# Half-height matmuls in pairs for a gated two-product layer: nine half passes in the first product, w_out stationary in the second, tiles of 1024 tokens

## What is computed

```python
# attention-like part: x (4, 4096, 192), weight_gen (4, 4096, 8 heads, 7 taps)
w = exp(weight_gen - max over taps);  w = w / (sum over taps + 1e-9)
x_pad = six zero rows ahead of each sequence
out[b, s, h, :] = sum over k of w[b, s, h, k] * x_pad[b, s + k, h, :]     # 24 channels per head
# feed-forward part, on x = out as (16384, 192); w_in (192, 2048), w_out (2048, 192)
h = x @ w_in
g = h * sigmoid(1.702 * h)
return g @ w_out                                                          # (16384, 192), float32
```

## Time and profile before

| what | us |
|---|---|
| median of 3 runs (1236.51 to 1236.57) | 1236.51 |
| the profiled execution's own time | 1236.58 |
| its span in the trace | 1234.8 |
| TensorE busy | 1189.4 (96%) |
| TensorE weight loads busy | 1071.5 (87%) |
| VectorE busy | 876.8 (71%) |
| ScalarE busy | 588.4 (48%) |
| first matmul starts | 36.32 |

### The profile page before, as it was taken

How to read it: one execution, slowest core, us unless ns; L and a number is a source line. 1 busy time by engine, 2 the same in 40 slices (tenths; PEclk the granted TensorE clock), 3 DMA queues, 4 the chain that set the end, 5 groups by cost and what they waited for, 6 DMA issues and landing times.

```text
span 1234.8 us, 17474 instructions
## 1 busy us (share of the span) xinstructions
PE 1189.4 (96%) x6656; PEld 1071.5 (87%) x6656; DVE 876.8 (71%) x1064; ACT 588.4 (48%) x726; POOL 34.2 (3%) x14
## 2 busy tenths in 40 slices
PE   0789999999999999999999999999999999999998
PEld 0678998998998998998998998998998998999998
DVE  7997777777777777777777777777777777777742
ACT  2467454454454454454454454454454454454453
POOL 5320000000000000000000000000000000000000
PEclk9999999999999999999999999999999999999999
DMA  6000000000000000000000000000000000000000
GB/s 273 18 7 25 31 31 30 30 14 16 30 30 30 30 15 15 30 30 30 30 15 16 30 30 30 30 17 14 30 30 30 30 17 14 30 30 30 14 14 13
DMA packets 10670, 37.43 MB, mean 30 GB/s; under 512 B 1312, under 2 KB 1568, under 8 KB 10528
## 3 DMA queue, kind: packets, MB, share of 16 engines
q1 hardware_dynamic: 10368, 36.18, 8.5%
q10 hardware_dynamic: 288, 1.05, 0.2%
HBM read 24.64 MB, written 12.58 MB: 30 GB/s over the span
## 4 chain that ended last, share of the span: by engine, by line
PE 92%; DVE 7%; DMA 1%; ACT 0%; issue 0%; SPq 0%; DVEq 0%
PE acc L411 31%; PE acc L413 15%; PE hid L392 10%; PE hid L393 9%; PE hid L395 9%; PE hid L394 9%; PE hid L396 9%; DVE prod L266 2%; DVE sums L271 1%; DVE gate_lo L333 1%; DVE tap_max L286 1%; DMA xwin<-in_x_runs 1%; DVE sums L266 0%; DVE conv L274 0%; DVE tap_norm L255 0%; DVE turned L297 0%
## 5 line engine op out<-in xcount | busy, mean ns | idle before, releaser
L411 PE MATMUL acc<-w,gate_hi 128*128 128x384 f32 x2048 | 601.0, 357 | 5.5 <-DVE gate_lo L333 4.8
L333 DVE TENSOR_TENSOR gate_lo<-gate,gate_hi 128x1024 fp32r<-128x1024 f32 x256 | 313.8, 1226 | 335.5 <-ACT gate_hi L219 335.5
L216 ACT ACTIVATE gate<-hid 128x1024 f32<-128x1024 f32 x256 | 262.7, 1026 | 604.0 <-PE hid L396 598.5
L413 PE MATMUL acc<-w,gate_lo 128*128 128x192 f32 x2048 | 519.1, 253 | 0.0
L411 PEld LDWEIGHTS acc<-w,gate_hi 128*128 128x128 f32 x2048 | 385.2, 188 | 18.7 <-DVE gate_lo L333 7.1
L413 PEld LDWEIGHTS acc<-w,gate_lo 128*128 128x128 f32 x2048 | 391.2, 191 | 10.7
L219 ACT ACTIVATE gate_hi<-hid 128x1024 fp32r<-128x1024 f32 x256 | 260.8, 1019 | 0.0
L392 PE MATMUL hid<-xt,w_hi 128*128 128x512 f32 x512 | 209.1, 408 | 36.3 <-DVE xt L306 36.3
L393 PE MATMUL hid<-xt,w_hi 128*128 128x512 f32 x512 | 204.7, 400 | 0.0
L395 PE MATMUL hid<-xt,w1r_hi 128*128 128x512 f32 x512 | 203.0, 396 | 0.0
L394 PE MATMUL hid<-xt,w_lo 128*128 128x512 f32 x512 | 202.8, 396 | 0.0
(11 more groups left out here) (27 smaller groups left out, 280.1 us busy)
## 6 DMA issues: line engine op xcount, KB each, us to landing
xwin<-in_x_runs SPq DMA_DIRECT2D x32, 528.0 KB, 3.8
out<-outs SPq DMA_DIRECT2D x32, 384.0 KB, 2.5
taps<-in_tap_runs SPq DMA_DIRECT2D x1, 3248.0 KB, 18.7
w_raw<-in_w_rows SPq DMA_DIRECT2D x2, 768.0 KB, 10.2
w_raw<-in_w_rows ACTq DMA_DIRECT2D x1, 512.0 KB, 4.1
w1r_raw<-in_w1r_rows ACTq DMA_DIRECT2D x1, 512.0 KB, 6.1
w_raw<-in_w_rows SPq DMA_DIRECT2D x1, 512.0 KB, 9.6
w1r_raw<-in_w1r_rows SPq DMA_DIRECT2D x1, 512.0 KB, 10.4
```

The lines of the kernel that those rows point to most:

```text
L216: nc.scalar.activation(gate[:, s, :], hid[:, s, :, :], ACT.Gelu_apprx_sigmoid).then_inc(gate_ready, 1)
L333: nc.vector.tensor_tensor(gate_lo[:, i, :], gate[:, m % 2, :], gate_hi[:, i, :], ALU.subtract).then_inc(gate_lo_ready, 1)
L411: nc.tensor.matmul(acc[:, t, 0:2 * D], gate_hi[:, i, g], w2[:, c, :], start=(c == 0), stop=False)
L413: last = nc.tensor.matmul(acc[:, t, D:2 * D], gate_lo[:, i, g], w2[:, c, 0:D], start=False, stop=(c == CH - 1))
```

## The change

**Tiles.** 64 runs instead of 32. A tile is 1024 tokens in two halves h of 512, and there are 16. 128 partitions hold half h (64 of them each), in it two groups of 96 channels by 32 runs. Each VectorE step of the convolution has 1536 elements a partition for 1024 tokens instead of 768 for 512. After one transposition (three slices k of 32 channels) the channels of half h are on partitions 64h to 64h+63, 64 at a time.

**First product.** A unit is one chunk of 128 hidden columns for each half, 16 units a tile, 256 in all. It makes 3 terms by 3 slices, nine passes; each pass is two matmuls of 64 x 128 weights by 512 tokens, one for each half of the array's rows. The halves' weights come from the upper or lower 64 partitions, and each partition half has at first only half of w_in's columns; four DMAs copy them across before unit 8 of tile 0.

**Second product.** w_out is stationary, the gate moves with 512 columns. The accumulators hold 128 output columns (`acc_main`) and the other 64, hi in the lower and lo in the upper half (`acc_rest`), for each h a bank. A chunk's 128 hidden columns are two half heights, and a bank may take only one half of the array at a time: rows 0-63 go to bank 0 while rows 64-127 go to bank 1 (straight), then the reverse (crosswise), with waits on TensorE's own semaphores at the turns. That is ten passes of two matmuls a unit.

**Around it.** Read-out is one copy each on ScalarE and VectorE for `acc_main`, then ScalarE copies and VectorE adds twice for `acc_rest`, in slot `v == 1`, on VectorE ahead of that unit's `gate_lo`. The output leaves in two stores a tile. `xwin` and the output buffers are single. GpSimd has no work: w_in's and w_out's lo parts and the taps' subtraction are VectorE's. The raw weights lie in the space of the later taps, so these are loaded only after the weights are split.

```diff
+CONV_AT = (4, 0, 2, 1, 1, 2, 1, 1, 2, 1, 1, 1, 0, 0, 0, 0)
+TURN_AT, ROUND_AT, SPLIT_AT = 11, 12, 13
+TAPS_AT = (1, 3, 6, 8)
...
-        xwin = sb("xwin", [P, 2, WIN, CB])
+        xwin = sb("xwin", [P, WIN, CB])
...
             load_taps(0, 0, taps_loaded[0])
+            sp.dma_start(xwin[:], x_runs[:, 0:WIN, :]).then_inc(x_loaded, 16)
+            sp.dma_start(w1_raw, w1_rows).then_inc(w1_loaded, 16)
+            sp.dma_start(w2_raw, w2_rows).then_inc(w2_loaded, 16)
             load_taps(1, 1, taps_loaded[1])
+            sp.wait_ge(w1_hi_ready, 1)
+            sp.dma_start(w1_hi[lower, :, 1, :].bitcast(F32), w1_hi[upper, :, 0, :].bitcast(F32)).then_inc(w1_doubled, 16)
...
+            sp.wait_ge(w2_lo_ready, 2)
+            load_taps(2, 1 + PARTS, taps_loaded[2])
 
             def tile(j, b):
+                if not is_last(j):
                     wait(sp, conv_ready, j + 1)
+                    sp.dma_start(xwin[:], x_runs[:, bass.ds(U * (j + 1), WIN), :]).then_inc(x_loaded, 16)
+                wait(sp, main_out_act, j + 1)
+                wait(sp, main_out_dve, j + 1)
+                sp.dma_start(rows[0:P, :], outs_main[:].rearrange("p h n -> p (h n)")).then_inc(main_stored, 16)
+                wait(sp, rest_out, 2 * (j + 1))
+                sp.dma_start(rows[P:D, :], outs_rest[:].rearrange("p h n -> p (h n)")).then_inc(rest_stored, 16)
...
             def first_product(j, b, v):
                 wait(pe, gate_hi_ready, n - 1)
-                    nc.tensor.matmul(to, w1_hi[:, f], hi, start=True, stop=False)
-                    nc.tensor.matmul(to, w1_hi[:, f], lo, start=False, stop=False)
-                    nc.tensor.matmul(to, w1_lo[:, f], hi, start=False, stop=False)
-                    nc.tensor.matmul(to, w1r_hi[:, f], rest, start=False, stop=False)
-                    last = nc.tensor.matmul(to, w1r_lo[:, f], rest, start=False, stop=True)
+                terms = [(w, part, k) for w, part in ((w1_hi, 0), (w1_lo, 0), (w1_hi, 1)) for k in range(SLICES)]
+                for i, (w, part, k) in enumerate(terms):
+                    for h in range(2):
+                        rows = slice(h * HALF, (h + 1) * HALF)
+                        last = nc.tensor.matmul(hid[:, v % 2, h, :], w[rows, k, q, f], xt[rows, b, part, k, :],
+                                                start=(i == 0), stop=(i == len(terms) - 1))
                 last.then_inc(hid_ready, 1)
...
+                    for r in range(2):
+                        h = 1 - r if crossed else r
+                        rows = slice(r * HALF, (r + 1) * HALF)
+                        done = nc.tensor.matmul(acc[:, h, :], w2[rows, chunk[h], cols], g[rows, s, h, :],
+                                                start=start, stop=stop)
...
                 wait(pe, gate_lo_ready, n + 1)
+                wait(pe, main_added, n)
+                halves(acc_main, gate_hi, MAIN, False, first, False)
+                halves(acc_main, gate_hi, MAIN_LO, False, False, False)
+                halves(acc_main, gate_lo, MAIN, False, False, False).then_inc(main_straight, 1)
+                if first:
+                    wait(pe, rest_out, 2 * j)
+                wait(pe, rest_added, n)
+                halves(acc_rest, gate_hi, REST_COLS, True, first, False)
+                halves(acc_rest, gate_lo, REST_COLS, True, False, False).then_inc(rest_crosswise, 1)
+                wait(pe, main_straight, n + 1)
+                halves(acc_main, gate_hi, MAIN, True, False, False)
+                halves(acc_main, gate_hi, MAIN_LO, True, False, False)
+                halves(acc_main, gate_lo, MAIN, True, False, last_unit).then_inc(main_added, 1)
+                wait(pe, rest_crosswise, n + 1)
+                halves(acc_rest, gate_hi, REST_COLS, False, False, False)
+                halves(acc_rest, gate_lo, REST_COLS, False, False, last_unit).then_inc(rest_added, 1)
```

More of the change, by code:

```diff
@@ L133, in over_tiles, with is_first, is_last, tap_span @@
                 body(TILES - BODY + b, b)
-        def last_tile(j):
+        def is_first(j):
+            return isinstance(j, int) and j == 0
+        def is_last(j):
             return isinstance(j, int) and j == TILES - 1
+        def tap_span(first, last):
+            return slice(TAP_PARTS[first][0] * HB * K, TAP_PARTS[last][1] * HB * K)
         @block.sync
@@ L140, in load_taps @@
             def load_taps(first, last, s):
-                lo, hi = TAP_PARTS[first][0] * HB * K, TAP_PARTS[last][1] * HB * K
-                sp.dma_start(taps[:, lo:hi], tap_runs[:, lo:hi]).then_inc(s, 16)
+                sp.dma_start(taps[:, tap_span(first, last)], tap_runs[:, tap_span(first, last)]).then_inc(s, 16)
             load_taps(0, 0, taps_loaded[0])
-            sp.dma_start(signs[:], sign_rows).then_inc(signs_loaded, 16)
-            for j in range(2):
-                sp.dma_start(xwin[:, j, :, :], x_runs[:, j * U:j * U + WIN, :]).then_inc(x_loaded[j], 16)
+            sp.dma_start(xwin[:], x_runs[:, 0:WIN, :]).then_inc(x_loaded, 16)
@@ L225, in tile @@
-                    if m == SPLIT_AT and not last_tile(j):
+                    wait(act, rest_added, n - SLOTS + 1)
+                    nc.scalar.activation(gate_hi[:, v % SLOTS, :, :], hid[:, v % 2, :, :], ACT.Gelu_apprx_sigmoid
+                                         ).then_inc(gate_hi_ready, 1)
+                    if v == EVICT_AT and not is_first(j):
+                        lift(j - 1)
+                    if is_first(j) and v in TAPS_AT:
+                        exponentials(2 + TAPS_AT.index(v))
@@ L226, in tile @@
+                    if v == ROUND_AT and not is_last(j):
                         round_tile(j + 1, (b + 1) % BODY)
             over_tiles(act, tile)
-            lift_cross(TILES - 1, (TILES - 1) % BODY)
+            lift(TILES - 1)
         SOFTMAX_STEPS = 4
@@ L327, in tile @@
             def tile(j, b):
-                known = isinstance(j, int)
-                for m in range(PAIRS):
-                    n = j * PAIRS + m
+                for v in range(UNITS):
+                    n = j * UNITS + v
+                    if v == EVICT_AT and not is_first(j):
+                        evict(j - 1)
                     wait(dve, gate_hi_ready, n + 1)
-                    i = (b * PAIRS + m) % HI_SLOTS
-                    nc.vector.tensor_tensor(gate_lo[:, i, :], gate[:, m % 2, :], gate_hi[:, i, :],
-                                            ALU.subtract).then_inc(gate_lo_ready, 1)
-                    if m == LAG - 1 and not (known and j == 0):
-                        evict(j - 1, (b + 1) % BODY)
-                    if known and j == 0 and m in MAX_AT:
-                        maxima(2 + MAX_AT.index(m))
-                    ahead = 1 if m < SPLIT_AT else 2
-                    if not (known and j + ahead >= TILES):
-                        first = BEFORE + sum(CONV_AT[:m]) if m < SPLIT_AT else sum(CONV_AT[SPLIT_AT:m])
-                        for q in range(first, first + CONV_AT[m]):
-                            conv_step(dve, j + ahead, (b + ahead) % BODY, q)
-                    if m == TURN_AT and not last_tile(j):
@@ new lines, in tile @@
+                    nc.vector.tensor_tensor(gate_lo[:, v % SLOTS, :, :], gate[:, v % 2, :, :],
+                                            gate_hi[:, v % SLOTS, :, :], ALU.subtract).then_inc(gate_lo_ready, 1)
+                    if is_first(j) and v in TAPS_AT:
+                        maxima_and_shift(2 + TAPS_AT.index(v))
+                    if is_last(j):
+                        continue
+                    for q in range(sum(CONV_AT[:v]), sum(CONV_AT[:v + 1])):
+                        conv_step(dve, j + 1, q)
```

376 lines of the change are left out of this document (155 added, 221 removed).

## The result

The changed kernel takes 1222.49 us, median of 4 runs (1220.93 to 1224.67); the kernel before takes 1236.54. The ratio is 0.9888, 95% interval 0.987 to 0.9905: 14 us faster. The forecast was 34 us faster, 1203 us. The profiled execution has a span of 1219.0 us, and 1220.93 in all.

What follows compares the result with a forecast made beforehand. TensorE's instruction rate was taken as the bound. 38.1 first matmul + 1135.9 for 256 units + 12 opening + 10 jumps + 4.8 end = 1200.8 us span, plus 1.78 outside it: 1203 us; range 1185 to 1310, own case 1190 to 1230.

Steps and rivals of the forecast that it cites:

- The rate after the change: TensorE, steady part: 19 slots a unit at 0.2335 us each, 4.437 us a unit against 4.627 a pair before.
- Rival A: TensorE slots: each weight load costs its own 20 ns, a slot is 254 ns, 1303 us in all; chance 0.13.
- D: Rival, TensorE slots: the 20 ns between matmuls disappear, 213 to 220 ns a slot, 1104 to 1137 us; chance 0.10.
- E: Rival, TensorE: the halves don't run together, 2341 us, or a load cannot lie beside its own matmul, 1721; together 0.05.
- The turns: TensorE's waits between straight and crosswise and between units: 50 ns to spare at the tightest, costed at nothing.
- B: Rival, second product: the turns stall TensorE 0.1 to 0.2 us a unit, 1229 to 1254 us; chance 0.10.
- VectorE and the window: Window load and read-out ahead of `gate_lo`: window lands 4.6 to 7.6 us after issue; costed at nothing.
- C: Rival, tile starts: the window starves VectorE, 3 us in each of 15 tiles, 1248 us; chance 0.07.
- The opening: Start of the kernel: first matmul near 38.1 us, then 12 us for the low clock and waits in the first tiles.
- The loop's code: TensorE's 5 jumps back: new body not held, each waits for a fetch; 2 us each, 10 us, bounds 0 to 19.
- The end: From the last matmul's end to the span's: 4.8 us, against 3.6 in the kernel before.
- the likeliest case: The forecast's own case for the whole kernel: 1203 us, own range 1190 to 1230, chance 0.55.

Runs made afterwards that it cites:

- the short couples: Changed kernel with each first-product matmul cut in two of 256 columns, 1236.66 us, or in four of 128 columns, 1714.81 us; single runs.
- the exponentials later: Changed kernel with ScalarE's four exponentials of the large taps moved from units 1, 3, 6, 8 of tile 0 to 3, 5, 8, 10: 1209.86 us.
- the halves apart: Changed kernel with the first product's two loops swapped, all nine passes of half 0, then all nine of half 1: 1506.59 us, single run.

## Why the prediction was wrong

**The rate after the change: right.** A slot was to cost 0.2335 us and a unit 4.437; it is 4.424. The value was taken from the single matmul of 512 columns, and it holds for the couple. The loads were given room for the worse case, one behind the other, 214 of 233 ns, with 19 to spare; the short couples show that they run at once in about 0.11 us. Rival A, 20 ns for each load, did not happen, nor did D; E fell with the halves in step.

**The turns: right**, at nothing. No wait of TensorE for itself stands in the list; B fell.

**VectorE and the window: right.** The window landed 5.2 us after its issue, in the forecast's 4.6 to 7.6. VectorE waited 43.0 us for it in all, up to 3.4 us a tile, and TensorE never for `gate_lo` in the steady part: the lag of two units is the cover that was named. C fell.

**The opening: the step that failed.** The first matmul was right within 1.3 us (36.8), and so was GpSimd's part: the 13 convolution steps took 1.75 us each with GpSimd idle. The taps landed at 53.4, as put (53 to 56). What failed is the sentence on who waits: "2.3 us of waiting for `gate_lo` of unit 2". I had followed VectorE's queue only. Moving the large taps' work puts an exponential into ScalarE's queue behind each part, and ScalarE, held there, held the gates. TensorE waited 7.5, 2.1, 3.3 and 0.6 us for it, 13.6 in all, where the forecast had four waits for `gate_lo` with 7.0 together; the wait for the first gate, 2.2 us, was forecast (2.6). And twice TensorE went on at the lower clock, which the forecast had for the start only (some 2.4 us): without its waits the opening lost 8.4 us, and 4.1 with the exponentials later, where the clock did not fall. Measured 24.2 for 12; the later exponentials bring it to 9.9, so with VectorE's queue alone the term would have been 2 us too high.

**The loop's code: right mechanism, term half as large as it is.** The forecast was 2 us for each of 5 jumps with 19 us as its bound; measured 19.5. Two things were mis-sized. I had half a microsecond of queued matmuls and about 2.5 us for a fetch; the branch takes 3.3 to 3.6. And I had not costed the clock: behind three of the five jumps TensorE went on at the lower level, which cost 1.65 us each. Removing the loop gives back 19.2.

**The end** took 5.5 instead of 4.8.

The two terms together, 22 us, less 4 for the units and the first matmul, are the miss of 18 in the span. The range given for the likeliest case, 1190 to 1230, holds the measured time, but the size of the gain, 14 us for 34, did not come out.

## What to carry to other kernels

When a step moves, follow it through every in-order queue that it passes: ask of each engine what stands behind the instruction that will wait, as a wait for a DMA travels from VectorE to ScalarE to TensorE. Count the instructions of a loop's body on TensorE: here 862 cost nothing at a jump, and 1720 or more cost a branch of 3.3 to 3.8 us, which can be avoided by writing the loop out, or halved by placing the jump where two microseconds of work are queued, which here also kept the clock up. Two matmuls of half height run at once at the price of one, if they are neighbours in the queue.

## What the runs showed of the hardware

- The two halves' weight loads run at once: a couple of 128-column matmuls starts every 0.1115 us, its two loads 10 ns apart, where one load of all rows takes 0.11.
- TensorE does not keep the program's order between the halves: with the halves apart, a matmul of the free half starts ahead of earlier ones of the other (702.46 before 702.70), and a unit is 5.55 us instead of 6.54. The Trainium skill (TensorE: Matmul & The Clock Gate, Packing small matmuls) has matmuls start and end in the program's order; this trace shows another.
- What is lost between couples is not fixed: 20 ns at 512 columns, 13 at 256.
- The halves run either together (3 to 15 ns apart) or about 150 ns apart, which makes a unit 4.415 to 4.423 or 4.433 us. It can change within one execution, and the two groups of times of one kernel, 5.4 us apart, suggest that it differs between executions. What decides it stays open.
- A body of 1720 instructions is fetched anew in each turn, and the taken branch to it takes 3.3 to 3.8 us, where one to held code takes 0.21. TensorE works off what is queued meanwhile.
